# Attention and two gated layers on one core: a third score block in idle banks, two places for turned blocks, and x awaited chunk by chunk

## The reference

```
scores = (q @ k^T) / sqrt(64)             # 32 heads, q, k, v: 576 x 64
keep only scores >= rowmax - tau          # tau = 0.02
attn   = exp(scores - rowmax) / (sum + 1e-9)
o      = attn @ v                         # heads joined: x, 2304 tokens x 512
x1     = (h * clip(h + 3, 0, 6) / 6) @ moe_w_out,    h = x @ moe_w_in    (512 -> 2048 -> 512)
out    = (h * sigmoid(1.702 h)) @ moe2_w_out,        h = x1 @ moe2_w_in
```

## Time and profile before

| | us |
|---|---|
| runs of the kernel before | 1087.25, 1087.51, 1087.97 (median 1087.51) |
| the profiled execution | 1087.71 |
| its span in the trace | 1085.9 |
| PE busy, weight loads busy | 1054.3 (97%), 990.0 (91%) |
| DVE, ACT, POOL busy | 803.7, 601.3, 472.2 |

### The profile page before, as it was taken

How to read it: one execution, slowest core, us unless ns; L and a number is a source line. 1 busy time by engine, 2 the same in 40 slices (tenths; PEclk the granted TensorE clock), 3 DMA queues, 4 the chain that set the end, 5 groups by cost and what they waited for, 6 DMA issues and landing times.

```text
span 1085.9 us, 18118 instructions
## 1 busy us (share of the span) xinstructions
PE 1054.3 (97%) x6536; PEld 990.0 (91%) x6536; DVE 803.7 (74%) x1437; ACT 601.3 (55%) x1073; POOL 472.2 (43%) x557
## 2 busy tenths in 40 slices
PE   6888899999999999999999999999999999999998
PEld 5676799999999999999999999998898989898897
DVE  5989988787888888676775747887674798666561
ACT  5888886767777777644542516444351636334240
POOL 3566756555646464435451504155140507323050
PEclk8999999999999999999999999999999999999999
DMA  4446453536335452562224041432203043331302
GB/s 128 118 137 183 132 137 99 137 90 161 100 101 124 131 138 75 135 174 91 93 71 153 2 132 63 139 102 71 95 1 126 11 131 112 97 117 39 107 1 88
DMA packets 102824, 112.41 MB, mean 104 GB/s; under 512 B 28096, under 2 KB 81488, under 8 KB 102736
## 3 DMA queue, kind: packets, MB, share of 16 engines
q1 hardware_dynamic: 102432, 110.97, 35.5%
q10 hardware_dynamic: 304, 0.30, 0.1%
HBM read 78.12 MB, written 33.10 MB: 102 GB/s over the span
## 4 chain that ended last, share of the span: by engine, by line
PE 80%; DVE 11%; issue 4%; ACT 3%; DMA 2%; SPq 1%; POOL 1%; DVEq 0%; ACTq 0%
PE score L871 10%; PE score L831 10%; PE score L747 8%; PE mm L831 8%; PE mm L785 7%; PE mm L776 7%; PE tr L762 6%; PE mm L792 6%; PE tr L871 5%; PE tr L831 4%; PE score L869 3%; DVE prob L987 2%; PE score L792 2%; PE tr L869 2%; PE mm L869 2%
## 5 line engine op out<-in xcount | busy, mean ns | idle before, releaser
L1623 POOL TENSOR_TENSOR gd_lo<-act_ring,gd_hi 128x384 fp32r<-128x384 f32 x144 | 157.2, 1112 | 350.3 <-ACT gd_hi L1408 348.6
L1298 ACT ACTIVATE pt_hi<-tr 128x640 fp32r<-128x640 f32 x144 | 101.7, 706 | 95.5 <-PE tr L762 94.9
L1005 DVE TENSOR_TENSOR pt_lo<-tr,pt_hi 128x640 fp32r<-128x640 f32 x144 | 118.3, 822 | 11.0 <-ACT pt_hi L1298 9.9
L979 DVE TENSOR_REDUCE neg_max<-score 128x1 f32<-128x576 f32 x144 | 108.0, 751 | 22.2 <-PE score L747 18.6
L987 DVE SCALAR_TENSOR_TENSOR prob<-score,thresh,prob 128x576 f32<-128x576 f32 x144 | 116.3, 808 | 0.1
L1587 POOL TENSOR_SCALAR thresh<-neg_max,tau_abs 128x1 f32<-128x1 f32 x144 | 41.7, 290 | 171.2 <-DVE neg_max L979 170.8
L747 PE MATMUL score<-k_hi,q_sp 128*128 128x288 f32 x320 | 96.7, 318 | 17.0 <-DVE prob L987 16.4
L762 PE MATMUL tr<-ident,prob 128*128 128x128 f32 x720 | 105.3, 278 | 6.7 <-issue 4.4
L1293 ACT ACTIVATE prob<-score,neg_max 128x576 f32<-128x576 f32 x144 | 106.4, 739 | 7.6 <-DVE neg_max L979 7.3
L762 PEld LDWEIGHTS tr<-ident,prob 128*128 128x128 f32 x720 | 83.2, 142 | 17.5 <-issue 16.3
L747 PE MATMUL score<-k_lo,q_sp 128*128 128x288 f32 x320 | 90.8, 299 | 0.2 <-DVE k_lo L974 0.2
(11 more groups left out here) (195 smaller groups left out, 3143.7 us busy)
## 6 DMA issues: line engine op xcount, KB each, us to landing
pair_raw<-x_t_scratch SPq DMA_DIRECT2D x36, 384.0 KB, 3.9
q_raw<-in_qT SPq DMA_DIRECT2D x64, 144.0 KB, 2.8
k_raw<-in_kT SPq DMA_DIRECT2D x62, 144.0 KB, 2.9
raw_a<-in_w_out SPq DMA_DIRECT2D x48, 128.0 KB, 2.2
o_parts_scratch<-o_t SPq DMA_DIRECT2D x32, 160.0 KB, 1.8
x_t_scratch<-x_raw SPq DMA_DIRECT2D x8, 576.0 KB, 3.3
part_t_scratch<-y_out SPq DMA_DIRECT2D x8, 576.0 KB, 3.6
y_ring<-part_t_scratch SPq DMA_DIRECT2D x24, 192.0 KB, 2.6
```

The lines of the kernel that those rows point to most:

```text
L979: dve.tensor_reduce(neg_max[:, r:r + 1], score[:, g % 2, :, 0:HALF], AX.XY, ALU.max, negate=True).then_inc(max_done, 1)
L1005: dve.tensor_tensor(pt_place(pt_lo, x), turned_place(x), pt_place(pt_hi, x), ALU.subtract).then_inc(pt_lo_done, 1)
L1298: act.activation(pt_place(pt_hi, x), turned_place(x), ACT.Copy).then_inc(pt_hi_done, 1)
L1623: pool.tensor_tensor(gd_lo[:, u, c, :], act_ring[:, g % 3, :], gd_hi[:, u, c, :], ALU.subtract).then_inc(g_lo_done, 1)
```

## The change

Four edits.

1. `tr` and `mm` become one tensor of four banks, `tr_mm`. The third block's scores (g = 2) go to its last two banks (where `pv_out` and `mix_out` lie) instead of waiting for a place in `score`; blocks 3 and 4 move a place on and wait for mask(0) and mask(1), from block 5 on the waits are as they were. Rounds 0 and 1 each get 8 transposes of the identity behind their scores.
2. ACT makes the second head's k_hi and q_hi before exponent(0) and scales q between exponents 0 and 1; POOL takes `low_k(1)` between the first two thresholds.
3. Up to block 39 (`SINGLE` = 40) odd blocks are turned into `turned_q`, columns 896 to 1535 of the four banks, even ones into `turned_p`, columns 0 to 639. `turn(x)` waits for `low_turned(x - 2)`, and only its last transpose, the one in the bank that both places share, waits for `low_turned(x - 1)`. `pv_out` and `mix_out` change places.
4. The first piece of a mixed tile waits for x chunk by chunk. Tiles 6 and 7 first take chunks 0 to 2 of x for all four banks (36 matmuls), then the last chunk for each.

```diff
+    SINGLE = BATCH_SLOTS + LAG - 4
...
-        pv_out, mix_out = mm[:, 0, :], mm[:, 1, :]
-        turned_p = tr[:, :, :].rearrange("p a n -> p (a n)")[:, 0:WIDE]
+        tr_mm = ctx.enter_context(nc.psum_tensor("tr_mm", [P, 4, 512], F32))
+        tr, mm = tr_mm[:, 0:2, :], tr_mm[:, 2:4, :]
+        mix_out, pv_out = mm[:, 0, :], mm[:, 1, :]
+        turned_p = tr_mm[:, :, :].rearrange("p a n -> p (a n)")[:, 0:WIDE]
+        turned_q = tr_mm[:, :, :].rearrange("p a n -> p (a n)")[:, 1536 - WIDE:1536]
+        def score_place(g):
+            if g == 2:
+                return mm[:, :, 0:HALF]
+            return score[:, (g + (g > 2)) % 2, :, 0:HALF]
...
             def scores(g):
-                wait(pe, mask_done, g - 1)
+                if g > 2:
+                    pe.wait_ge(mask_done, g - 2 if g < 5 else g - 1)
...
             def turn(x):
                 pe.wait_ge(mask_done, x + 1)
-                wait(pe, pt_lo_done, x)
-                wait(pe, inv_copied, x // SLOTS)
-                for c in range(CHUNKS):
-                    m = pe.transpose(turned_p[:, c * P:c * P + P], ...)
+                place = turned_columns(x)
+                if x == 1:
+                    pe.wait_ge(mask_done, 3)
+                wait(pe, pt_lo_done, x - 1 if x < SINGLE else x)
+                order = (1, 2, 3, 4, 0) if place is turned_q else range(CHUNKS)
+                for c in order:
+                    if c == order[-1]:
+                        wait(pe, pt_lo_done, x)
+                        wait(pe, inv_copied, x // SLOTS)
+                    m = pe.transpose(place[:, c * P:c * P + P], ...)
...
             def mixed_piece(ti, p, begin, end):
-                        pe.wait_ge(x_lo_done, KC * (ti + 1))
...
-                    r = h_chunk(mix_out, p, range(begin, end))
+                    for k in range(begin, end):
+                        if p == 0:
+                            pe.wait_ge(x_lo_done, KC * ti + k + 1)
+                        r = h_chunk(mix_out, p, (k,))
...
             for g in range(END):
                 if g + 2 < G:
                     scores(g + 2)
+                if g < 2:
+                    for _ in range(8):
+                        pe.transpose(turned_p[:, 0:P], ident[:, :], ident[:, :])
...
             for ti in range(MIXED, TILES):
+                for k in range(KC - 1):
+                    pe.wait_ge(x_lo_done, KC * ti + k + 1)
+                    for c in range(len(h_bank)):
+                        h_chunk(h_bank[c], c, (k,))
                 pe.wait_ge(x_lo_done, KC * (ti + 1))
                 for c in range(FC):
                     if c >= len(h_bank):
                         pe.wait_ge(mm_drained, base + c - len(h_bank) + 1)
-                    h_chunk(h_bank[c % len(h_bank)], c).then_inc(mm_filled, 1)
+                        h_chunk(h_bank[c % len(h_bank)], c).then_inc(mm_filled, 1)
+                    else:
+                        h_chunk(h_bank[c], c, (KC - 1,)).then_inc(mm_filled, 1)
...
-            exponent(0)
-            exponent(1)
             high_k(1)
             high_q(1)
+            exponent(0)
             scale_q(1)
+            exponent(1)
...
             threshold(0)
+            low_k(1)
             threshold(1)
-            low_k(1)
             low_q(1)
```

More of the change, by code:

```diff
@@ L255, in attention_moe_kernel @@
         score = ctx.enter_context(nc.psum_tensor("score", [P, 2, 2, 512], F32))
-        tr = ctx.enter_context(nc.psum_tensor("tr", [P, 2, 512], F32))
-        mm = ctx.enter_context(nc.psum_tensor("mm", [P, 2, 512], F32))
-        pv_out, mix_out = mm[:, 0, :], mm[:, 1, :]
-        turned_p = tr[:, :, :].rearrange("p a n -> p (a n)")[:, 0:WIDE]
+        tr_mm = ctx.enter_context(nc.psum_tensor("tr_mm", [P, 4, 512], F32))
[3 more added lines that the diff above has]
+        turned_q = tr_mm[:, :, :].rearrange("p a n -> p (a n)")[:, 1536 - WIDE:1536]
         turned_inv = tr[0:SLOTS, 1, 2 * P:3 * P]
+        def score_place(g):
+            if g == 2:
+                return mm[:, :, 0:HALF]
+            return score[:, (g + (g > 2)) % 2, :, 0:HALF]
         y_bank = [score[:, 0, 0, :], score[:, 0, 1, :], score[:, 1, 0, :], score[:, 1, 1, :]]
@@ L359, in pt_place, with turned_columns @@
                            ap=[list(base.ap[0]), list(base.ap[1]), [after.offset - base.offset, 2], list(base.ap[2])])
+        def turned_columns(x):
+            return turned_q if x < SINGLE and x % 2 else turned_p
         def turned_place(x):
             if kind(x) != MID:
-                return turned_p.rearrange("p (c n) -> p c n", c=CHUNKS)
-            return turned_p.rearrange("p (c h n) -> p c h n", c=CHUNKS, h=2)
+                return turned_columns(x).rearrange("p (c n) -> p c n", c=CHUNKS)
+            return turned_columns(x).rearrange("p (c h n) -> p c h n", c=CHUNKS, h=2)
         def group_last(n):
@@ L746, in scores @@
                             pe.wait_ge(first_k_lo_done, 1)
-                        m = pe.matmul(score[:, g % 2, half, 0:HALF], q_sp[:, col:col + P],
+                        m = pe.matmul(score_place(g)[:, half, :], q_sp[:, col:col + P],
                                       k_part[:, side, half * HALF:half * HALF + HALF],
@@ L758, in turn @@
                 pe.wait_ge(mask_done, x + 1)
-                wait(pe, pt_lo_done, x)
-                wait(pe, inv_copied, x // SLOTS)
-                for c in range(CHUNKS):
-                    m = pe.transpose(turned_p[:, c * P:c * P + P], prob[:, x % PROBS, c * P:c * P + P], ident[:, :])
+                place = turned_columns(x)
[7 more added lines that the diff above has]
+                        wait(pe, inv_copied, x // SLOTS)
+                    m = pe.transpose(place[:, c * P:c * P + P], prob[:, x % PROBS, c * P:c * P + P], ident[:, :])
                 m.then_inc(turned, 1)
@@ L766, in prob_v @@
                 k, side = n % 4, (n % 4) // 2
+                if n == 0 and not low:
+                    pe.wait_ge(mask_done, 3)
                 width = GROUP_COLS[k][1]
@@ L798, in mixed_piece @@
                 if p < FC:
+                    if p == 0 and begin == 0:
+                        pe.wait_ge(pt_lo_done, SINGLE)
                     if p == 0:
-                        pe.wait_ge(x_lo_done, KC * (ti + 1))
                         pe.wait_ge(w_lo_done, 2 * UNITS)
@@ L978, in row_max @@
                 dve.wait_ge(scores_ready, g + 1)
-                dve.tensor_reduce(neg_max[:, r:r + 1], score[:, g % 2, :, 0:HALF], AX.XY, ALU.max,
+                dve.tensor_reduce(neg_max[:, r:r + 1], score_place(g), AX.XY, ALU.max,
                                   negate=True).then_inc(max_done, 1)
@@ L986, in mask @@
                 p = prob[:, g % PROBS, 0:S].rearrange("p (a n) -> p a n", a=2)
-                dve.scalar_tensor_tensor(out=p, in0=score[:, g % 2, :, 0:HALF], scalar=thresh[:, r:r + 1], in1=p,
+                dve.scalar_tensor_tensor(out=p, in0=score_place(g), scalar=thresh[:, r:r + 1], in1=p,
                                          op0=ALU.is_ge, op1=ALU.mult, accum_out=total[:, g // SLOTS % 2, kind(g):kind(g) + 1]
@@ L1292, in exponent @@
                 wait(act, turned, g - PROBS + 1)
-                act.activation(prob[:, g % PROBS, 0:S].rearrange("p (a n) -> p a n", a=2), score[:, g % 2, :, 0:HALF],
+                act.activation(prob[:, g % PROBS, 0:S].rearrange("p (a n) -> p a n", a=2), score_place(g),
                                ACT.Exp, bias=neg_max[:, r:r + 1]).then_inc(exp_done, 1)
```

## The result

| | before | after |
|---|---|---|
| median of 6 runs each, us | 1087.22 (1084.92 to 1087.97) | 1078.52 (1078.30 to 1078.72) |
| span of the profiled execution | 1085.9 | 1076.7 |
| PE, DVE, ACT, POOL busy | 1054.3, 803.7, 601.3, 472.2 | 1046.8, 802.8, 601.6, 473.2 |

What follows compares the result with a forecast made beforehand. PE bounds the kernel from 140 us on, DVE is fullest from 21 to 120, and before 21 a relay with no engine full. Terms 4.4 + 1.7 + 0.5 + 0.2 + 0 - 0.5 = 6.3 us gave 1081.2, range 1078.4 to 1084.8.

Steps and rivals of the forecast that it cites:

- two places: Up to block 39: turns end about 0.4 us sooner, cutting DVE's 5.1 us of waits; gain 1.7 us, between 0 and 5.1.
- the spell at 77 us: Low TensorE clock around blocks 27 and 28, costing 1.1 us; may go, stay or move: 0.5 gain, between 1.1 and -1.1.
- The head: Start of the kernel: block 4's row maximum at 14.4 us instead of 18.79; gain 4.4 us, between 2.7 and 4.5.
- the clock falls at the head all the same: Rival: TensorE's clock still drops at the head, which gains only 2.7 us; 1082.9 us in all, chance 0.15.
- From block 5 on the waits are the old ones, and blocks run at the old pace.: Behind the head: waits and pace of blocks stay as before, so blocks run 4.4 us earlier.
- its last rival: Slower: PE works in shorter bursts and its clock falls again and again; 1094.4 us with 12 such rounds, chance 0.03.
- The three late rounds: Attention rounds where ACT reaches the high part late and DVE waits 0.5 to 0.57 us: 3 x 0.4 = 1.2 us gain.
- The mixed start: PE's 0.53 us wait for x's last chunk goes, but the next scores need a late mask: 0.2 gain, 0 to 0.5.
- Tile 6: Starts 0.5 us earlier but gives it back, as its fifth matmul group cannot start sooner: 0, from -0.3 to 0.5.
- The wait of 0.6 us before the fifth group: Sign in tile 6: a start without a wait, then PE waits about 0.6 us before the fifth group of matmuls.
- Tile 7: Gates start 1.0 us later and PE waits 0.5 us for g's last low part: -0.5, between 0 and -1.0.
- more than forecast: Rival: two places return 3.4 us, the spell at 77 us goes, tile 7 waits for nothing; 1078.0 us, chance 0.09.

Runs made afterwards that it cites:

- e5: The changed kernel with edit 2 undone (second head's splits behind exponent(1) on ACT and threshold(1) on POOL again): 1080.10 us, ratio 0.9935.
- e4: The changed kernel without the 16 transposes of the identity in rounds 0 and 1: 1078.65 us, ratio 0.9926.
- e6: The kernel before with only transposes of the identity added, 16 ahead of the loop and 16 behind the scores of rounds 0 and 1: 1083.20 us, ratio 0.9965.
- e9: The changed kernel with edit 4 undone and without the 16 added transposes: 1078.51 us, ratio 0.9921.
- e3: The kernel before with edit 4 alone, keeping the new order of waits in `turn`: 1088.06 us, ratio 1.0014.
- e2: The kernel before with edit 3 alone (two places for turned blocks up to block 39): 1082.57 us, ratio 0.9962.
- e1: The changed kernel with one place for turned blocks and x awaited whole, leaving edits 1 and 2 and the new order of waits in `turn`: 1081.22 us, ratio 0.9949.
- e11: The changed kernel again, without an edit, in a later series: 1078.37 us, ratio 0.9917.
- e10: e6 with two places for turned blocks (edit 3) added: 1081.70 us, ratio 0.9948.
- e12: The kernel of e8 repeated in another series, without a further edit: 1077.43 us, ratio 0.9914.
- e8: The changed kernel with edit 4 undone altogether, x awaited whole in the mixed stage and tiles 6 and 7: 1077.57 us, ratio 0.9910.
- e7: The changed kernel with x whole again in tile 7, only tile 6 keeping the chunks outermost: 1077.80 us, ratio 0.9914.

## Why the prediction came out as it did

The direction and the mechanism came true; the time lies at the lower end of the range because two terms were too small (two places, the spell at 77 us) and a third was missing (the spell at 20 us).

- **The head, 4.4 us.** Measured 4.45 (block 4 at 14.26, 14.4 forecast). The replay of the relay holds, and e5 shows that the splits' new order carries 1.5 of it; what it would bring without the third place was not run. e4, with the clock up at 1.00 and no added transposes, gains as much. What the replay could not tell was that 1.5 of these 4.45 are clock (e6). The rival "the clock falls at the head all the same" was wrong for after, but e9 is that rival: 1.0 us at block 7, of which 8 x (0.24 - 0.135) = 0.84 are the score matmuls, the price that the prediction had put at 1.1. Its head still gains 3.64 at block 4, more than the lower end of 2.7.
- **"From block 5 on the waits are the old ones, and blocks run at the old pace."** This is the step that failed. The waits were the old ones; the pace was not. The clock of before was still 0.75 from 20.3 to 27 us, a stretch that the prediction had no row of (its last rival counts three falls before 81 us, its sum prices two), and it cost 1.2 us (blocks 4 to 7: 5.63 - 4.45; the same in e6, 2.68 - 1.50).
- **The spell at 77 us, 0.5.** The whole of it went: the interval between the row maxima of blocks 27 and 28 is 2.37 us instead of 3.65. Where it is missing with one place, that round takes 2.48 (e3) and 2.44 (e6) and the next some 0.2 more than in before, so about 1.0 of the gain is the spell and 0.3 the two places. What removes it is open. It is gone in all profiled runs with edit 3 (e2, after and the others) and is there in e1 (clock 0.85), but it is gone in e3 too, which has neither the second place, nor the earlier start, nor the transposes of e6.
- **Two places, 1.7.** 2.7 in after (9.37 at block 47 in e11, less 5.64 and the spell's 1.0) and 2.9 in e10 against e6. DVE's waits for ACT fell from 5.1 to 0.7. The three late rounds gave 0.35, 0.30 and 0.30, together 0.95 where 1.2 was counted; the other rounds gave more than the 0.5 allowed for them, so the scores' path did not replace all of their waits. The largest single piece, 0.76, is for the most part no wait for ACT: the round from block 37 takes 2.58 or 2.6 us in every kernel with two places and 3.33 or 3.34 in every one without. In before a small operation of DVE stands beside an addition of POOL there and takes 0.74 us, in after the two do not meet and it takes 0.28 (timelines of before and after):

```profile
105.90 0.80 POOL L1596 TENSOR_TENSOR x_raw<-x_raw,x_low 128x288 f32<-128x288 f32 x1
...
105.99 0.74 DVE L994 TENSOR_SCALAR total_e<-total 128x9 f32<-128x9 f32 x1
...
97.01 0.28 DVE L1036 TENSOR_SCALAR total_e<-total 128x9 f32<-128x9 f32 x1
```

- **The mixed start, 0.2.** Nothing (e12): the scores behind the piece wait for a mask in any case (0.37 us, at 121.97). The chunk-wise waits of the later tiles, counted at nothing, cost 0.2 to 0.3 us, in steps of 0.11 at the start of a tile (e12).
- **Tile 6, 0.** The last row maximum starts 8.50 us earlier than in before (438.29), the first matmul 9.07 (462.58), DVE's first product 9.09 (468.48), the fifth group 9.14 (468.98). So 0.6 is gained at the start and kept, not given back; but not by edit 4: in e8, which has x whole, the first matmul of tile 6 also starts 24.3 us after the last row maximum. The edit's own term is 0 as forecast, for another reason than forecast. The wait of 0.6 us before the fifth group, which was to show the step right, did not come: the gates start as soon as the first bank is full, 5.36 us after the first matmul, and 48 matmuls last 6.4. But the start has no wait in e8 and e12 either, where x is waited for whole; the 0.5 us of before were gone because the low part of the last chunk of x starts 23.6 (after, e8) or 23.9 us (e12) after the last row maximum instead of 24.3.
- **Tile 7, -0.5.** -0.7 (e7). The chain was read rightly (gates 1.0 later, last low part of g 1.0 later, PE waits at number 34 of the second product, 33 forecast); only the size was off.

Of the rivals, "more than forecast" (1078.0) came nearest. Its two places (3.4) were too many and its tile 7 wrong, and it lacked the spell at 20 us. In sum, along the profiled run: 4.45 + 1.2 + 1.3 (blocks 27 to 28) + 2.2 (other rounds) is 9.1 at block 47; from there to the last row maximum 0.7 are lost (0.3 by edit 4; the other 0.4 in the rounds named under e3), 0.1 up to the first dense matmul (0.6 of x gained, 0.7 of tile 7 lost), and 0.8 more are in the dense stage; 9.1 of 9.2 us of span. The 0.8 is not the change's: the profiled run of before loses 0.2 at 732.7 us and 0.6 at 773.3, where PE waits (timeline), and e3 and e6, with the same dense code, lose neither.

```profile
773.30 0.41 PE L831 MATMUL mm<-xs_hi,ws_a 128*128 128x384 f32 x1 [0.34 <-DVE y_ring L1121]
```

Block 5's row maximum is at 16.64 (17 forecast), and the first mixed matmul 9.9 us earlier, not 6.
